# Turning the scaled k with VectorE's 32x32 blocks and DMAs, instead of TensorE transposes, from the third chunk on

## The reference

```python
for t in range(S):
    cur = np.einsum('bhd,bhe->bhde', u[None] * kt, vt)
    y[:, :, t] = np.einsum('bhd,bhde->bhe', rt, state + cur)
    state = wt[:, :, :, None] * state + np.einsum('bhd,bhe->bhde', kt, vt)
...
h = x @ w_in;  g = np.where(h > 0, h, np.exp(np.minimum(h, 0)) - 1);  x = g @ w_out
...
p = domain_probs / (domain_probs.sum(-1, keepdims=True) + 1e-09)
for e in range(E):
    out += p[:, e:e + 1] * (np.maximum(x @ w1[e], 0.0) @ w2[e])
```

## Time and profile before

| what | value |
|---|---|
| median of 3 runs | 649.91 us (649.89 to 650.03) |
| the profiled execution's own time | 649.99 us |
| its span on the core | 648.1 us |
| busy: PE, DVE, ACT, POOL | 642.3, 413.5, 243.0, 295.4 us |
| granted TensorE clock, mean | 0.999 of full speed |

### The profile page before, as it was taken

How to read it: one execution, slowest core, us unless ns; L and a number is a source line. 1 busy time by engine, 2 the same in 40 slices (tenths; PEclk the granted TensorE clock), 3 DMA queues, 4 the chain that set the end, 5 groups by cost and what they waited for, 6 DMA issues and landing times.

```text
span 648.1 us, 13433 instructions
## 1 busy us (share of the span) xinstructions
PE 642.3 (99%) x4884; PEld 596.3 (92%) x4884; DVE 413.5 (64%) x778; ACT 243.0 (37%) x569; POOL 295.4 (46%) x370
## 2 busy tenths in 40 slices
PE   8999999999999999999999999999999999999998
PEld 5999999887788888999999999999999999999997
DVE  7888888865357667656565656565656565656564
ACT  4786656655345554322222222222222222222221
POOL 5897323420399999997019900019900019000000
PEclk9999999999999999999999999999999999999999
DMA  8932233200000133100013100013100011001011
GB/s 328 403 149 89 88 126 135 86 1 2 2 2 0 50 98 99 49 2 1 1 50 97 50 2 0 0 50 98 50 1 0 0 50 49 1 1 49 0 50 49
DMA packets 13281, 38.11 MB, mean 59 GB/s; under 512 B 1968, under 2 KB 4016, under 8 KB 13232
## 3 DMA queue, kind: packets, MB, share of 16 engines
q1 hardware_dynamic: 12944, 37.03, 16.1%
q10 hardware_dynamic: 288, 0.39, 0.2%
HBM read 35.06 MB, written 2.36 MB: 58 GB/s over the span
## 4 chain that ended last, share of the span: by engine, by line
PE 90%; POOL 5%; DVE 2%; issue 1%; DMA 1%; SPq 0%; ACT 0%; POOLq 0%; DVEq 0%
PE bank L1312 29%; PE bank L1313 29%; PE bank L1314 28%; POOL w_lo L524 4%; PE bank L1160 1%; PE bank L1227 1%; DMA rkw<-rkw_dram 1%; PE bank L1171 1%; PE bank L1239 1%; PE bank L1183 0%; POOL tok L501 0%; POOL tok L505 0%; PE bank L1247 0%; PE bank L1243 0%; DVE fr L847 0%
## 5 line engine op out<-in xcount | busy, mean ns | idle before, releaser
L1312 PE MATMUL bank<-x_lo,w_hi 128*128 128x256 f32 (+2 forms) x416 | 137.9, 332 | 0.3 <-DVE x_lo L934 0.2
L1313 PE MATMUL bank<-x_hi,w_lo 128*128 128x256 f32 (+2 forms) x416 | 135.2, 325 | 0.0
L1314 PE MATMUL bank<-x_hi,w_hi 128*128 128x256 f32 (+2 forms) x416 | 135.2, 325 | 0.0
L1313 PE MATMUL bank<-w_hi,g_lo 128*128 128x384 f32 x384 | 129.6, 338 | 0.0
L1314 PE MATMUL bank<-w_hi,g_hi 128*128 128x384 f32 x384 | 129.3, 337 | 0.0
L1312 PE MATMUL bank<-w_lo,g_hi 128*128 128x384 f32 x384 | 129.0, 336 | 0.0
L810 ACT ACTIVATE g_hi<-bank 128x512 fp32r<-128x512 f32 x96 | 57.5, 598 | 144.3 <-DVE bank L1027 122.4
L1312 PEld LDWEIGHTS bank<-x_lo,w_hi 128*128 128x128 f32 x416 | 78.3, 188 | 8.8 <-issue 0.4
L1314 PEld LDWEIGHTS bank<-x_hi,w_hi 128*128 128x128 f32 x416 | 78.2, 188 | 7.4
L1313 PEld LDWEIGHTS bank<-x_hi,w_lo 128*128 128x128 f32 x416 | 78.3, 188 | 7.1
L1020 DVE TENSOR_TENSOR u_sum<-p_copy,bank 128x256 f32<-128x256 f32 x56 | 23.6, 421 | 92.4 <-ACT p_copy L732 91.8
(11 more groups left out here) (134 smaller groups left out, 1269.2 us busy)
## 6 DMA issues: line engine op xcount, KB each, us to landing
raw<-w_dram SPq DMA_DIRECT2D x48, 384.0 KB, 3.7
rkw<-rkw_dram SPq DMA_DIRECT2D x10, 772.5 KB, 4.5
tok<-tok_dram SPq DMA_DIRECT2D x10, 576.0 KB, 5.6
out_dram<-acc SPq DMA_DIRECT2D x10, 192.0 KB, 1.9
rkw<-rkw_dram SPq DMA_DIRECT2D x2, 512.0 KB, 4.8
rkw<-rkw_dram SPq DMA_DIRECT2D x2, 260.5 KB, 3.1
tok<-tok_dram SPq DMA_DIRECT2D x2, 192.0 KB, 6.0
out_dram<-acc ACTq DMA_DIRECT2D x2, 192.0 KB, 1.9
```

The lines of the kernel that those rows point to most:

```text
L1312: pe.matmul(out, wh, ml, start=start, stop=False, skip_group_check=shared)
L1313: pe.matmul(out, wl, mh, start=False, stop=False, skip_group_check=shared)
L1314: return pe.matmul(out, wh, mh, start=False, stop=stop, skip_group_check=shared)
```

## The change

For chunks 2 to 9 TensorE's transposes and ScalarE's copy go. VectorE's `transpose` turns every 32x32 block of the scaled k (128 partitions, 512 columns) in one instruction into a new buffer `k_blocks`, where each block lies turned but in the partition group of its head rows. SP then issues 16 DMAs of 32 partitions by 128 columns (16 KB each) from `k_blocks` to `kt_sb`, which put the blocks in the partitions of their tokens. `update` waits for all 16 and picks its columns by another stride. Chunks 0 and 1 stay as they were.

```diff
+TURNS = {c: step for c, step in SCALE_K.items() if c < NC - B}
+LATE_TURNS = {c: SCORES[c] for c in TILE_STARTS if FIRST < c < NC - B}
+MOVED = 16 * STRIPS_P * STRIPS_P
...
             def load_rkw(c):
                 need(sp, s_py, c - DEEP + 1)
-                need(sp, s_pkt, min(c - DEEP + 1, NUPDATE))
+                need(sp, s_kb, c - DEEP + 1 - FIRST)
...
+            def move_blocks(c):
+                sp.wait_ge(s_kb, c + 1 - FIRST)
+                sp.wait_ge(s_pu, c)
+                for d in range(STRIPS_P):
+                    for t in range(STRIPS_P):
+                        sp.dma_start(kt_sb[t * STRIP:(t + 1) * STRIP, d * P:(d + 1) * P],
+                                     k_blocks[d * STRIP:(d + 1) * STRIP, t, :]).then_inc(s_moved, 16)
...
             for c in range(4, NC):
                 load_rkw(c)
                 load_tok(c)
+                move_blocks(c - 2)
...
-                    if c < NUPDATE:
-                        copy_kt(c, BESIDE)
...
+            def turn_blocks(c):
+                dve.wait_ge(s_kp, c + 1)
+                need(dve, s_moved, MOVED * (c - FIRST))
+                dve.transpose(k_blocks[:, :, :].rearrange("q t (a j) -> q t a j", a=PAIRS),
+                              raw_k(c).rearrange("q (a t i) -> q t a i", a=PAIRS, i=STRIP)).then_inc(s_kb, 1)
...
                 for c in due(n, -1):
                     bonus(c)
+                for c in due(n, 0, LATE_TURNS):
+                    turn_blocks(c)
                 for c in due(n, 0, PRODUCTS):
                     products(c)
...
                 for c in due(n, 0, SCALE_K):
                     scale_k(c)
+                for c in due(n, 0, TURNS):
+                    turn_blocks(c)
...
             def update(c, banks):
-                pe.wait_ge(s_kt, c + 1)
+                if c < FIRST:
+                    pe.wait_ge(s_kt, c + 1)
+                else:
+                    pe.wait_ge(s_moved, MOVED * (c + 1 - FIRST))
...
+                        first = p * P + STRIP * i if c < FIRST else i * P + STRIP * p
                         ins = pe.matmul(banks["u"][rows, p * D:(p + 1) * D],
-                                        kt_sb[:, p * P + STRIP * i:p * P + STRIP * i + STRIP], v[:, h * D:(h + 1) * D],
+                                        kt_sb[:, first:first + STRIP], v[:, h * D:(h + 1) * D],
...
             def y_free(c):
-                pe.wait_ge(s_kt, min(c + 1, NUPDATE))
+                pe.wait_ge(s_kt, FIRST)
                 pe.wait_ge(s_x, c)
...
                 for c in due(n, 0):
                     scores(c, BESIDE)
-                    if c < NUPDATE:
-                        turn_k(c, BESIDE)
```

More of the change, by code:

```diff
@@ L106 @@
 STRIPS = DM // STRIP
+STRIPS_P = P // STRIP
+MOVED = 16 * STRIPS_P * STRIPS_P
 PIECES = 2
@@ L168, in bass_linear_attention_elu_ffn_dense_experts @@
             kt_sb = sb("kt_sb", [P, PAIRS * P], scope=scope)
+            k_blocks = sb("k_blocks", [P, STRIPS_P, PAIRS * STRIP], scope=scope)
             att = sb("att", [P, 2, PAIRS, CH], scope=scope)
@@ L245, in bass_linear_attention_elu_ffn_dense_experts @@
         s_kt = sem("s_kt")
+        s_kb = sem("s_kb")
+        s_moved = sem("s_moved")
         s_att = sem("s_att")
@@ L1165, in turn_k @@
                 pe.wait_ge(s_kp, c + 1)
-                if banks is BESIDE:
-                    pe.wait_ge(s_x, c)
                 k = k_of(c)
```

## The result

The changed kernel takes 673.57 us (median of 5 runs, 672.45 to 673.59) against 649.93 us for the kernel before (649.89 to 650.15): a ratio of 1.0359, with a 95% interval from 1.0347 to 1.0371, slower by 23.6 us. The forecast was 655.0 with a range to 661.0. The sign was right, the size was not: of the loss, only a fifth had been seen.

What follows compares the result with a forecast made beforehand. TensorE was taken to bound the kernel, busy 99%, though not on the chain of waits up to 61.39 us. +4.6 - 1.2 + 1.65 + 0.4 - 0.4 = +5.0 us on 649.99 gave 655.0, range 649.8 to 661.0.

Steps and rivals of the forecast that it cites:

- What TensorE's transposes are worth: TensorE: dropping the transposes gains 0.41 us a chunk, 2.5 us for six chunks, nothing for chunks 2 and 3.
- What VectorE gets: Block transposes on VectorE: 0.60 us each, ending after 0.68; chunk 2's makes scores of chunk 4 start 0.35 us later.
- What SP gets: SP's 16 issues a chunk, 0.48 us apart, 1.9 us to land: a move of 9.2 us, bounds 6.1 to 12.0.
- Chunks 2, 3, 5, 6 and 7: Updates there: no wait for moves; room 0.5 us at chunk 2, 1.3 to 1.7 at chunks 5 to 7.
- Chunks 4 and 8: Updates of the chunks turned late wait for their moves: net 4.6 us at chunk 4, 1.65 at chunk 8.
- Rival B: SP's move is slower than 10.6 us, through long issues or 0.59 us each; with 12.0, 663.3 us; chance 0.20.
- Rival D: All SP moves hidden, needing a move under 4.3 us; sum -1.1 us, 648.9, down to 646.7; chance 0.11.
- Behind 172 us: Sign: the forecast is wrong if TensorE is late somewhere behind 172 us, where nothing was changed.

Runs made afterwards that it cites:

- the removal alone: The changed kernel without turns and moves, still without TensorE's transposes from chunk 2 on; update reads what chunk 1 left in kt_sb: 647.87 us, ratio 0.9967.
- the kernel with four issues: The changed kernel with the same 256 KB a chunk in 4 DMAs of 128 partitions in place of 16, blocks not in their right places: 648.83 us.
- the last experiment: The changed kernel with SP's 16 moves of chunk c-2 ahead of the two loads of chunk c: 669.66 us, ratio 1.0311.
- the additions alone: The kernel before plus VectorE's turns and SP's 16 DMAs of 16 KB a chunk to DRAM, which nothing waits for: 650.81 us, ratio 1.0012.

## Why the prediction was wrong, point by point

**What TensorE's transposes are worth.** Right. 2.5 us forecast for six chunks, 2.1 measured by the removal alone, and with nothing for chunks 2 and 3.

**What VectorE gets.** Right. 0.71 us for a turn, against 0.68 taken; scores of chunk 4 came 0.31 us later in the kernel with four issues, 0.35 forecast. Eight turns and the issues cost 0.8 us without a waiter.

**What SP gets.** Here it failed. "I take the second, 0.48 rounded": the issue is 0.59 us long and comes every 0.63. Fifteen steps are 9.5 us, not 7.2, and long issues add up to 0.9. From the turn's end the move took 11.3 us at the least (chunk 4), 12.8 at chunk 2 and 14.3 at chunk 7, not 9.2. The landing, 1.8, was right in the median and at chunks 4, 6 and 8; the last move of chunk 2, whose own issue was a long one, took 2.56, and that of chunk 7 took 3.68. The 0.1 us to wake SP stood in no row; SP's first issue of chunk 4 started 0.02 us after the turn. The two spacings in the trace were of large loads, 0.59 and 0.49, and the first was discarded because of its crowd. The difference of 0.15 looks small; it was multiplied by fifteen, and then fell on room of 0.5 to 1.7 us per chunk.

**Chunks 2, 3, 5, 6 and 7.** "No wait" was wrong, and it followed from the step above: a move of 12.8 us is 3.6 over the forecast's, the room was 0.5, which leaves 3.1, and 3.04 were measured. Two long issues in that burst make 1.4 of it. For the others the prediction placed the burst behind the token load, but it did not ask what happens once a chunk is late: update, load, burst and landing up to the next update form a ring of 13.0 to 13.6 us, 15.1 with chunk 7's late landing, and TensorE's 12.0 cannot catch up in it.

**Chunks 4 and 8.** The mechanism was right and undersized: 5.66 and 4.65 us of waiting, against some 5 and 2 us. VectorE's `turn_blocks` for 5 and 9 did wait for the same DMAs (6.9 us the longest).

**TensorE's clock.** Not in the forecast at all, nor in its bounds. 8.1 us were lost at half the clock behind four waits of 2.9 us and more. Filling the waits with work won only 2.5 of them, since SP's pace came to light beneath and the filling itself was in the way once.

**Rival B** had a move of 12.0 us, within the 11.3 to 14.3 measured, and gave 663.3. Its own items add up to +14.3 and not +13.3, so it should have said 664.3. It still missed 9 us, for it had neither the waits of chunks 2 and 3 in its sum nor the ring or the clock. The range ended at 661.0, so even the sum of B, the case with the right mechanism, lay outside it. **Rival D** came true when its condition was met: 648.83 us with four issues, 648.9 forecast. Its condition was put wrongly: a move under 4.3 us, with the forecast's own 0.1 and 1.9, leaves (4.3 - 2.0)/15 = 0.15 us an issue and not 0.25. Fewer issues met it, not shorter ones.

**Behind 172 us** of the old time nothing changed, as forecast: of the 23.7 us by which the span grew, 23.6 were lost before the scores of chunk 11.

## What to carry to other kernels

Count DMAs before bytes: a burst of small ones costs its issues in a row on one queue, and here that time, not bandwidth, stood between the last producer and the first reader. When a transfer's latency comes near the period of the loop that it serves, add up the whole ring (reader, release, issue, landing) and compare it with the period: past that point every turn is late, not only the tight ones. Where a price is multiplied by the count of a burst, take the upper end of its rows, for a small error in it becomes a large one. Price a wait on the bounding engine with what it may do to that engine's clock. And before a run is taken as a sign of a theory, look whether the time was won where the theory says: the last experiment's was not.

## What the runs showed of the hardware

- One SP issue of a DMA within SBUF takes 0.59 to 0.60 us in the median for 16, 32 and 64 KB alike, 0.63 from one to the next. Issues of 16 KB from SBUF to DRAM took 0.42 in the median (the additions alone); loads from DRAM had taken 0.33 behind a wait and 0.49 in a row when calm. So the price differs with the kind of DMA and, from 16 to 64 KB, not with its bytes; why is open.
- Single issues of 1.1 to 2.0 us occur in all of these kernels, before the change too. What they are stays open.
- A move of 16 KB lands 1.8 us after its issue in the median, but up to 4.5. The last of a burst, on which `update` waits, took 1.8 in five bursts of the changed kernel and 2.5 to 3.7 in three. What makes them late stays open.
- A write of 256 KB to DRAM lands in 2.0 us alone and in 6.4 us behind 1.35 MB of loads.
- Behind waits of TensorE of 2.9 to 5.7 us in the changed kernel its granted clock was 0.50 for some 3 to 6 us; behind one of 1.4 us it stayed at 1.00. With chunks 4 and 8 back on TensorE it was 0.50 behind waits of 2.25 and 3.42 us and 1.00 behind one of 3.00. With products in the waits it stayed at 1.00.
- VectorE turns 128x512 float32 in 32x32 blocks in 0.71 us, as fast as it multiplies them.
